# Attention scores of the last step, moved behind the next group of turns

## The chip, the cores and the metric

The kernel runs on one core of a Trainium2 chip. The metric is the device time of one execution in microseconds (us), from inputs in the chip's memory to the output in it. A core has a matrix engine (TensorE, in the rows PE for its matmuls and PEld for its weight loads), a vector engine (VectorE, DVE), a scalar engine (ScalarE, ACT), GpSimd (POOL) and an engine that issues transfers (SyncE, SP). Each of them runs its own instructions in the order in which the program gives them, and waits on semaphores for the others.

## What is computed

An attention layer, a dense layer pair and a routed layer pair, one after the other. The change lies in the attention, so its reference stands here; the other two follow on its output of 2304 x 512.

```python
batch, n_heads, seq, head_dim = (4, 8, 576, 64)

def _attn_ref(q, k, v):
    B, H, S, D = q.shape
    block = 64
    scores = (1.0 / np.sqrt(D)) * np.matmul(q, k.transpose(0, 1, 3, 2))
    pos = np.arange(S)
    mask = pos[:, None] // block >= pos[None, :] // block
    scores = np.where(mask, scores, -1000000000.0)
    scores = scores - np.max(scores, axis=-1, keepdims=True)
    attn = np.exp(scores)
    attn = attn / (np.sum(attn, axis=-1, keepdims=True) + 1e-09)
    return np.matmul(attn, v).astype(np.float32)
```

## The kernel before

The 32 heads are worked on in 16 pairs (`PAIRS`, index `u`), two heads side by side in the 128 partitions. The 576 rows of a head are nine blocks of 64; block `i` needs the first `64*(i+1)` keys. The nine blocks of a pair are taken in four steps, `STEPS = [(8, 5), (4, 3), (7, 6), (2, 1, 0)]`. Steps 0 and 2 use the first two banks of the score memory `s_ps`, steps 1 and 3 the other two, so that step `n` may be written only when the exponentials of step `n - 2` have read theirs.

For one step the engines do this in turn:

- PE `score(u, j)`: the products of queries and keys (L1320, 64 rows by 64 columns of the array, two heads at a time).
- DVE `most(u, j)`: the largest score of each row, one reduction per block (L902). It waits for `scored`.
- ACT `exp(u, j)`: the exponentials with their row sums, one ACTIVATE per block (L703). It waits for `maxed`.
- DVE `invert(u, j)`: adds 1e-9 to the row sums (L907), takes the reciprocal (L909) and, for steps 0 to 2, multiplies the step's first block (L914). It waits for `exped` of the whole step. POOL `normalise(u, j)` multiplies the other blocks (L558).
- PE `turn_first(u, j)` and `turn_second(u, j)`: transposes of the probabilities (L1291), the first into the bank `a_ps`, the second into `d_ps`.
- ACT `first_out(u, j)` (L684) copies `a_ps` and DVE `second_out(u, j)` (L896) copies `d_ps` into `pt`. Each of the two banks holds one group of turns at a time: the next group into `d_ps` waits for `dve_free`, the next into `a_ps` for `act_free`.
- PE `weigh_many(u, ...)` and `weigh_few(u)`: the products with the values (L1342), the second for blocks 0 to 3. ACT `many_x` and `few_x` (L684) copy them out.

The rows of keys and queries of pair `u + 1` are turned by `turn_keys` and `turn_queries` (L1273) through the same two banks, and copied out by `keys_out` on ACT and `queries_out` on DVE (L888).

The order on each engine is written out by hand in a loop over `u`, and pairs overlap: while the scores of pair `u` are made, the last two steps of pair `u - 1` are turned and weighed. On PE one round of the loop is: scores 0 of `u`; turns of step 2 of `u - 1`; scores 1; first part of keys and queries of `u + 1`; first part of `weigh_many(u - 1)`; turns of step 3 of `u - 1`, mixed with the rest of keys and queries; scores 2; rest of `weigh_many(u - 1)`; turns of step 0 of `u`; scores 3; `weigh_few(u - 1)`; turns of step 1. On DVE a round begins with `invert(u - 1, 3)`, which stands in front of `most(u, 0)`, `second_out(u - 1, 2)` and `most(u, 1)`. In the last round there are no keys and queries to turn; after it PE turns step 2 of pair 15, waits for the exponentials of its step 3 (their banks are needed), and starts on the dense layers (`hidden`, L1372), whose first inputs `x_hi` and `x_lo` come from ACT (L684) and DVE (`split_x`, L924, queued behind `invert(15, 3)`).

Of the kernel before, what the change touches and what calls it, by code (L numbers as in the profile page):

```python
# [27 lines left out]
def routed_transformer_block(  # L28
# [101 lines left out]
    def blocks_before(u, j):  # L130

        return NB * u + sum(len(c) for c in STEPS[:j])
# [147 lines left out]
    with ctx:  # L280
# [74 lines left out]
        def scores(i):  # L355
            return s_ps[:, SCORE_AT[i]:SCORE_AT[i] + BLK * (i + 1)]
# [6 lines left out]
        def x_at(u):  # L363
            return u % PPB * TOK + u // PPB * SEQ
# [317 lines left out]
        def _(act):  # L682
            def high(dst, src):
                return act.activation(dst, src, ACT.Copy)  # L684


            def keys_out(u, n):
                act.wait_ge(act_full, A_TURN["k", u, n])
                high(kt[:, u % 2, TURNED[n]:TURNED[n + 1]],
                     a_ps[:, TURN_AT[n]:TURN_AT[n] + TURNED[n + 1] - TURNED[n]]).then_inc(act_free, 1)  # L690

            def first_out(u, j):
                cs = first_turn(j)
                at = slot(cs[0][0], 0)

                act.wait_ge(act_full, A_TURN["k", u + 2, 1] if j == 3 and u + 2 < PAIRS else A_TURN["p", u, j])
                high(pt[:, u % 2, at:at + len(cs), :].rearrange("p c n -> p (c n)"), a_ps[:, 0:P * len(cs)]).then_inc(act_free, 1)

            def exp(u, j):
                for m, i in enumerate(STEPS[j]):  # L700

                    act.wait_ge(maxed, blocks_before(u, j) + {8: 2, 1: 3}.get(i, m + 1))
                    act.activation(probs[:, PROB_AT[i]:PROB_AT[i] + BLK * (i + 1)], scores(i), ACT.Exp,  # L703
                                   bias=neg_max[:, i:i + 1], accum_out=row_sum[:, j, m:m + 1]).then_inc(exped, 1)
# [5 lines left out]
            def few_x(u):  # L710
                act.wait_ge(few_done, u + 1)
                high(x_t[:, x_at(u):x_at(u) + BLK * FEW], o_few).then_inc(few_out, 1)
# [15 lines left out]
            for u in range(PAIRS):  # L728
                more = u + 1 < PAIRS
                if u > 0:  # L730
                    first_out(u - 1, 2)
                exp(u, 0)
                if more:
                    keys_out(u + 1, 0)
                exp(u, 1)
                if u > 0:
                    first_out(u - 1, 3)
                if more:
                    keys_out(u + 1, 1)
                else:  # L740

                    act.wait_ge(dve_full, D_TURN["q", u, 1])
                    split_x(0, parts=range(0, 2))
                exp(u, 2)
                if u > 0:
                    many_x(u - 1)
                first_out(u, 0)
                exp(u, 3)
                first_out(u, 1)
                if u > 0:  # L750
                    few_x(u - 1)
            u = PAIRS - 1
            first_out(u, 2)
            split_x(0, parts=range(2, KC))
# [122 lines left out]
        def _(dve):  # L877
# [13 lines left out]
            def second_out(u, j):  # L891
                cs = second_turn(j)
                at = [slot(i, c) for i, c, _ in cs]
                step = at[1] - at[0]
                dve.wait_ge(dve_full, D_TURN["q", u + 2, 1] if j == 3 and u + 2 < PAIRS else D_TURN["p", u, j])
                dve.tensor_copy(pt[:, u % 2, at[0]:at[-1] + 1:step, :],  # L896
                                d_ps[:, 0:P * len(cs)].rearrange("p (c n) -> p c n", n=P)).then_inc(dve_free, 1)

            def most(u, j):
                dve.wait_ge(scored, NST * u + j + 1)  # L900
                for i in STEPS[j]:
                    dve.tensor_reduce(neg_max[:, i:i + 1], scores(i), AX_X, ALU.max, negate=True).then_inc(maxed, 1)  # L902

            def invert(u, j):
                n = len(STEPS[j])
                dve.wait_ge(exped, exps(u, j))
                dve.tensor_scalar(row_sum[:, j, 0:n], row_sum[:, j, 0:n], 1e-9, None, ALU.add).then_inc(summed, 1)  # L907
                dve.wait_ge(summed, NST * u + j + 1)
                dve.reciprocal(row_inv[:, j, 0:n], row_sum[:, j, 0:n]).then_inc(inverted, 1)  # L909
                if j < NST - 1:  # L910
                    dve.wait_ge(inverted, NST * u + j + 1)
                    i = STEPS[j][0]
                    p = probs[:, PROB_AT[i]:PROB_AT[i] + BLK * (i + 1)]
                    dve.tensor_scalar(p, p, row_inv[:, j, 0:1], None, ALU.mult).then_inc(long_normed, 1)  # L914
# [13 lines left out]
            for u in range(PAIRS):  # L928
                more = u + 1 < PAIRS
                if u > 0:  # L930
                    invert(u - 1, 3)
                most(u, 0)
                if u > 0:
                    second_out(u - 1, 2)
                most(u, 1)
                if more:
                    queries_out(u + 1, 0)
                invert(u, 0)
                if u > 0:
                    second_out(u - 1, 3)  # L940
                    if more:
                        queries_out(u + 1, 1)
                most(u, 2)
                if more and u == 0:
                    queries_out(u + 1, 1)
                invert(u, 1)
                second_out(u, 0)
                most(u, 3)
                invert(u, 2)
                second_out(u, 1)  # L950
            invert(PAIRS - 1, 3)

            dve.wait_ge(few_out, PPB)
# [302 lines left out]
        def _(pe):  # L1256
# [46 lines left out]
            def turn_second(u, j):  # L1303
                dve_bank(D_TURN["p", u, j])
                pe.wait_ge(short_normed, pool_normed(u, j))
                turn_probs(j, second_turn(j), d_ps).then_inc(dve_full, 1)

            def score(u, j):

                n = NST * u + j  # L1310
                if n >= 2:
                    pe.wait_ge(exped, exps((n - 2) // NST, (n - 2) % NST))
                if j == 0:
                    pe.wait_ge(act_free, A_TURN["k", u, 1])
                    pe.wait_ge(dve_free, D_TURN["q", u, 1])
                def product(m, i, lo, hi):
                    for h in range(2):
                        own = slice(BLK * h, BLK * h + BLK)
                        g = h if m == 0 else 1 - h
                        mm = pe.matmul(scores(i)[BLK * g:BLK * g + BLK, lo:hi], qt[own, u % 2, BLK * i:BLK * i + BLK],  # L1320
                                       kt[own, u % 2, lo:hi], start=True, stop=True, skip_group_check=True)
                    return mm

                if j == 0:

                    product(1, 5, 0, BLK * 6).then_inc(five_scored, 1)
                    product(0, 8, 0, 512)
                    pe.wait_ge(five_scored, u + 1)
                    mm = product(0, 8, 512, SEQ)
                else:  # L1330
                    for m, i in enumerate(STEPS[j]):
                        mm = product(m, i, 0, BLK * (i + 1))
                mm.then_inc(scored, 1)
# [84 lines left out]
            for u in range(PAIRS):  # L1418
                more = u + 1 < PAIRS
                score(u, 0)  # L1420
                if u > 0:
                    turn_first(u - 1, 2)
                    turn_second(u - 1, 2)
                score(u, 1)
                if more:
                    turn_keys(u + 1, 0)
                    turn_queries(u + 1, 0)
                if u > 0:
                    weigh_many(u - 1, (0, 1))
                    turn_first(u - 1, 3)  # L1430
                    if more:
                        turn_keys(u + 1, 1)
                    turn_second(u - 1, 3)
                    if more:
                        turn_queries(u + 1, 1)
                score(u, 2)
                if more and u == 0:
                    turn_keys(u + 1, 1)
                    turn_queries(u + 1, 1)
                if u > 0:  # L1440
                    weigh_many(u - 1, (2, 3, 4))
                turn_first(u, 0)
                turn_second(u, 0)
                score(u, 3)
                if u > 0:
                    weigh_few(u - 1)
                turn_first(u, 1)
                turn_second(u, 1)
            u = PAIRS - 1
            turn_first(u, 2)  # L1450
            turn_second(u, 2)
# [192 lines left out]
```

## Time and profile before

| | us |
|---|---|
| median of 3 runs | 793.68 |
| lowest and highest | 793.31 and 795.92 |
| the profiled execution | 793.63 |
| its span in the profile | 791.9 |

The profiled execution took 793.63 us, 1.7 us more than its span; that remainder lies outside the instructions. PE is counted busy in 98% of the span, DVE in 63%, ACT in 37%, POOL in 32%. The attention takes the first 190 us, the dense layers come next, and the routed layers last. The granted clock of TensorE is given in shares of 2.4 GHz.

In a row of the timeline the columns are: start in us, busy us, engine, line, operation, what is written and what is read, form and count; in brackets the idle time of the engine just before and who ended it. Rows of the same form that follow each other are merged, and the us are then those of all of them together.

### The profile page before, as it was taken

To read this page: it belongs to the slowest core of one execution; us is meant where nothing else is said; L and a number is where in the kernel's file an instruction comes from. 1 tells how busy PE (TensorE), PEld (TensorE's weight loads), DVE (VectorE), ACT (ScalarE), POOL (GpSimd) and SP (SyncE) were. 2 spreads that over 40 slices of the span, in tenths; PEclk is the share of its full clock that TensorE was granted. 3 is DMA by queue.
4 is the path that set the end of the run, shared out by engine and by line. 5 is a ranking of instruction groups with operands and counts; after the bars stand their busy time and mean duration, and the time that the engine had idled before them with its cause. 6 is when DMAs were issued, how large, how long until landed. Compare 5 with 4: busy or idle time off the path is not lost.

```text
span 791.9 us, 14922 instructions
## 1 busy us (share of the span) xinstructions
PE 774.8 (98%) x4600; PEld 605.9 (77%) x4601; DVE 501.6 (63%) x1242; ACT 296.3 (37%) x738; POOL 252.0 (32%) x307
## 2 busy tenths in 40 slices
PE   5999999999999999999999999999999999999996
PEld 3565556555888888888888888888998888888885
DVE  4887888876543376665766566654558565666653
ACT  3676767675101121113011220112217264555642
POOL 4767677776870000002000200002131223333333
PEclk9999999999999999999999999999999999999999
DMA  8243454321337330001000010000172376655564
GB/s 183 75 99 92 103 118 113 87 72 36 109 78 2 53 122 0 1 1 54 0 0 0 0 54 1 0 1 1 54 192 88 123 241 203 201 211 193 178 212 148
DMA packets 88154, 69.27 MB, mean 87 GB/s; under 512 B 66962, under 2 KB 66962, under 8 KB 88104
## 3 DMA queue, kind: packets, MB, share of 16 engines
q1 hardware_dynamic: 83160, 62.93, 29.7%
q0 software_dynamic: 3760, 5.38, 2.1%
q8 instruction: 30, 0.49, 0.3%
q10 hardware_dynamic: 1184, 0.30, 0.2%
q14 instruction: 20, 0.16, 0.1%
HBM read 62.97 MB, written 8.84 MB: 91 GB/s over the span
## 4 chain that ended last, share of the span: by engine, by line
PE 73%; DMA 14%; issue 5%; DVE 3%; POOL 2%; POOLq 1%; SPq 0%; DVEq 0%
PE psum L1372 50%; DMA xg<-out_dram,rec_next 8%; PE psum L1320 7%; PE psum L1342 6%; PE psum L1291 6%; DMA out_dram<-y_rows,rec_now 4%; PE psum L1273 2%; DMA out_dram<-y_rows,rec_early 2%; POOL rec_next L629 1%; PE psum L1468 1%; DMA q_rows<-in_q_dram 1%; DVE neg_max L902 1%; DVE we L1219 1%; POOLq L395 0%; POOL probs L558 0%
## 5 line engine op out<-in xcount | busy, mean ns | idle before, releaser
L800 ACT ACTIVATE g<-psum 128x512 f32<-128x512 f32 (+1 forms) x80 | 44.5, 556 | 306.8 <-PE psum L1372 306.8
L1106 DVE TENSOR_TENSOR g<-psum,g 128x512 f32<-128x512 f32 (+1 forms) x80 | 51.0, 638 | 157.6 <-ACT g L800 157.4
L583 POOL DMA_INDIRECT lists<-rec,slot_i x18 | 19.2, 1069 | 331.5 <-DVE slot_i L1040 327.5
L558 POOL TENSOR_SCALAR probs<-probs,row_inv 128x384 f32<-128x384 f32 (+2 forms) x96 | 99.0, 1042 | 57.1 <-DVE row_inv L909 57.1
L1372 PE MATMUL psum<-x_hi,wi_hi 128*128 128x512 f32 x256 | 100.1, 391 | 0.0
L1372 PE MATMUL psum<-x_hi,wi_lo 128*128 128x512 f32 x256 | 99.7, 389 | 0.0
L1372 PE MATMUL psum<-x_lo,wi_hi 128*128 128x512 f32 (+1 forms) x256 | 99.6, 389 | 0.0
L703 ACT ACTIVATE probs<-psum,neg_max 128x576 f32<-128x576 f32 (+2 forms) x144 | 74.6, 526 | 34.4 <-DVE neg_max L902 33.0
L1136 DVE TENSOR_TENSOR we<-w_half,we x96 | 59.0, 685 | 33.3 <-ACT we L684 33.3
L1372 PE MATMUL psum<-wo_hi,g_hi 128*128 128x512 f32 x192 | 74.9, 390 | 0.1
L1372 PE MATMUL psum<-wo_lo,g_hi 128*128 128x512 f32 x192 | 74.7, 389 | 0.0
L1372 PE MATMUL psum<-wo_hi,g_lo 128*128 128x512 f32 x192 | 74.7, 389 | 0.0
L684 ACT ACTIVATE we<-w_half (+1 forms) x112 | 60.1, 620 | 30.9 <-PE psum L1559 27.7
L902 DVE TENSOR_REDUCE neg_max<-psum 128x1 f32<-128x576 f32 (+2 forms) x144 | 62.9, 484 | 13.5 <-PE psum L1320 13.4
L1554 PE MATMUL psum<-we,xe_hi 128*128 (+1 forms) x240 | 61.0, 396 | 0.0
L1320 PE MATMUL psum<-kt,qt 64*64 64x64 f32 (+7 forms) x640 | 59.7, 435 | 0.8 <-DVE qt L888 0.5
L1579 PE MATMUL psum<-we,he_hi 128*128 (+1 forms) x240 | 58.8, 397 | 0.5 <-DVE y_rows L1202 0.5
L1342 PE MATMUL psum<-pt,v_rows 128*64 128x320 f32 (+4 forms) x448 | 56.1, 370 | 0.4 <-DVE pt L896 0.4
L1110 DVE TENSOR_TENSOR g_lo<-g,g_hi 128x512 fp32r<-128x512 f32 (+1 forms) x80 | 54.7, 683 | 2.8
L1372 PEld LDWEIGHTS psum<-x_hi,wi_lo 128*128 128x128 f32 x256 | 48.1, 188 | 10.1
L1372 PEld LDWEIGHTS psum<-x_hi,wi_hi 128*128 128x128 f32 x256 | 48.1, 188 | 10.0 <-issue 0.2
L1372 PEld LDWEIGHTS psum<-x_lo,wi_hi 128*128 128x128 f32 x256 | 48.1, 188 | 9.8
(229 smaller groups left out, 1486.7 us busy)
## 6 DMA issues: line engine op xcount, KB each, us to landing
w_half<-in_moe_w_dram SPq DMA_DIRECT2D x64, 512.0 KB, 3.8
q_rows<-in_q_dram SPq DMA_DIRECT2D x32, 144.0 KB, 3.0
out_dram<-x_rows SPq DMA_DIRECT2D x18, 256.0 KB, 2.1
k_rows<-in_k_dram SPq DMA_DIRECT2D x30, 144.0 KB, 3.2
v_rows<-in_v_dram SPq DMA_DIRECT2D x32, 128.0 KB, 2.3
w_raw<-in_moe_w_in_dram SPq DMA_DIRECT2D x16, 256.0 KB, 3.5
w_raw<-in_moe_w_out_dram SPq DMA_DIRECT2D x16, 256.0 KB, 2.6
wide_x<-w_rows SPq DMA_DIRECT2D x4, 256.0 KB, 5.3
```

The source lines that it names most:

```text
L558: pool.tensor_scalar(p, p, row_inv[:, j, m:m + 1], None, ALU.mult).then_inc(short_normed, 1)
L684: return act.activation(dst, src, ACT.Copy)
L703: act.activation(probs[:, PROB_AT[i]:PROB_AT[i] + BLK * (i + 1)], scores(i), ACT.Exp, bias=neg_max[:, i:i + 1], accum_out=row_sum[:, j, m: ...
L902: dve.tensor_reduce(neg_max[:, i:i + 1], scores(i), AX_X, ALU.max, negate=True).then_inc(maxed, 1)
L1106: dve.tensor_tensor(g_f, h_at(f, first, last), g_f, ALU.subtract).then_inc(g_done, 1)
L1110: dve.tensor_tensor(g_at(g_lo, f, last), g_f, g_at(g_hi, f, last), ALU.subtract).then_inc(g_lo_done, 1)
L1136: ins = dve.tensor_tensor(lo, w_half[:, bass.ds(h % 2, 1), cols].rearrange("p o n -> p (o n)"), hi, ALU.subtract)
L1320: mm = pe.matmul(scores(i)[BLK * g:BLK * g + BLK, lo:hi], qt[own, u % 2, BLK * i:BLK * i + BLK], kt[own, u % 2, lo:hi], start=True, stop=T ...
L1342: mm = pe.matmul(dst[own, :], v_rows[0:k, u % 2, c, own], pt[0:k, u % 2, at:at + step * (n - 1) + 1:step, own], start=first, stop=last, sk ...
L1372: mm = pe.matmul(dst, w, m, start=(first and n == 0), stop=(last and n == 2), skip_group_check=True)
L1554: pe.matmul(dst, xe_hi[:, kk, :], weights(h, part, F2 * kk + 512 * n), start=(kk == part == 0), stop=False, skip_group_check=True)
L1579: pe.matmul(y_ps, he_hi[:, t, :], weights(h, part, DM * t), start=(t == part == 0), stop=False, skip_group_check=True)
```

## The change

The group of step 3 (its scores on PE, its row maxima on DVE, its exponentials on ACT) is moved for all pairs but the first. On PE it stood between the turns of step 0 and `weigh_few`; now it stands behind the turns of step 1, directly in front of the next round's scores 0. On DVE `most(u, 3)` moves behind `invert(u, 2)` and `second_out(u, 1)`, directly in front of the next round's `invert(u, 3)`. On ACT `exp(u, 3)` moves behind `first_out(u, 1)` and `few_x(u - 1)`, directly in front of the next round's `first_out(u, 2)`. POOL's and SP's code is as before, and no instruction is added or taken away.

```diff
@@ ACT
                 first_out(u, 0)
-                exp(u, 3)
+                if u == 0:
+                    exp(u, 3)
                 first_out(u, 1)
                 if u > 0:
                     few_x(u - 1)
+                    exp(u, 3)
@@ DVE
                 second_out(u, 0)
-                most(u, 3)
+                if u == 0:
+                    most(u, 3)
                 invert(u, 2)
                 second_out(u, 1)
+                if u > 0:
+                    most(u, 3)
@@ PE
                 turn_second(u, 0)
-                score(u, 3)
-                if u > 0:
+                if u == 0:
+                    score(u, 3)
+                else:
                     weigh_few(u - 1)
                 turn_first(u, 1)
                 turn_second(u, 1)
+                if u > 0:
+                    score(u, 3)
```

PE before, from the turns of step 0 of a pair to the next pair's first scores (L1291 turns, L1320 scores, L1342 products with the values):

```order
L1291 MATMUL psum<-ident,probs 128x128 x4
L1291 MATMUL psum<-swap,probs 128x128 x3
L1291 MATMUL psum<-ident,probs 64x128
L1320 MATMUL psum<-kt,qt 64x192 x2
L1320 MATMUL psum<-kt,qt 64x128 x2
L1320 MATMUL psum<-kt,qt 64x64 x2
L1342 MATMUL psum<-pt,v_rows 64x256 x2
L1342 MATMUL psum<-pt,v_rows 64x128 x2
L1291 MATMUL psum<-ident,probs 128x128 x3
L1291 MATMUL psum<-swap,probs 128x128 x2
L1320 MATMUL psum<-kt,qt 64x384 x2
L1320 MATMUL psum<-kt,qt 64x512 x2
```

The same place after the change (lines are five higher):

```order
L1296 MATMUL psum<-ident,probs 128x128 x4
L1296 MATMUL psum<-swap,probs 128x128 x3
L1296 MATMUL psum<-ident,probs 64x128
L1347 MATMUL psum<-pt,v_rows 64x256 x2
L1347 MATMUL psum<-pt,v_rows 64x128 x2
L1296 MATMUL psum<-ident,probs 128x128 x3
L1296 MATMUL psum<-swap,probs 128x128 x2
L1325 MATMUL psum<-kt,qt 64x192 x2
L1325 MATMUL psum<-kt,qt 64x128 x2
L1325 MATMUL psum<-kt,qt 64x64 x2
L1325 MATMUL psum<-kt,qt 64x384 x2
L1325 MATMUL psum<-kt,qt 64x512 x2
```

The scores of 192, 128 and 64 columns, those of step 3, now stand next to the scores of 384 and 512 columns, those of the next pair's step 0.

DVE before, from the copy of step 0's turns to the copy of step 2's turns in the next round (the reductions x3 are step 3's, those x2 the next pair's step 0):

```order
L896 COPY pt<-psum 128x512
L902 TENSOR_REDUCE neg_max<-psum 128x1 x3
L907 TENSOR_SCALAR row_sum<-row_sum 128x2
L909 RECIPROCAL row_inv<-row_sum 128x2
L914 TENSOR_SCALAR probs<-probs,row_inv 128x512
L896 COPY pt<-psum 128x256
L907 TENSOR_SCALAR row_sum<-row_sum 128x3
L909 RECIPROCAL row_inv<-row_sum 128x3
L902 TENSOR_REDUCE neg_max<-psum 128x1 x2
L896 COPY pt<-psum 128x512
```

The same place after the change (lines are two higher):

```order
L898 COPY pt<-psum 128x512
L909 TENSOR_SCALAR row_sum<-row_sum 128x2
L911 RECIPROCAL row_inv<-row_sum 128x2
L916 TENSOR_SCALAR probs<-probs,row_inv 128x512
L898 COPY pt<-psum 128x256
L904 TENSOR_REDUCE neg_max<-psum 128x1 x3
L909 TENSOR_SCALAR row_sum<-row_sum 128x3
L911 RECIPROCAL row_inv<-row_sum 128x3
L904 TENSOR_REDUCE neg_max<-psum 128x1 x2
L898 COPY pt<-psum 128x512
```

Step 3's three reductions now stand directly in front of L909 on three columns, which waits for the exponentials of the same step.

## Rows read from the trace of the kernel before

**Rows 1.** The page, busy time of each engine, and the chain that ended last.

```profile
PE 774.8 (98%) x4600; PEld 605.9 (77%) x4601; DVE 501.6 (63%) x1242; ACT 296.3 (37%) x738; POOL 252.0 (32%) x307
...
PE 73%; DMA 14%; issue 5%; DVE 3%; POOL 2%; POOLq 1%; SPq 0%; DVEq 0%
```

**Rows 2.** Busy time in one round (stretch; PE, PEld, DVE, ACT, POOL; clock, DMA, GB/s).

```profile
107.06:118.22 11.16, 11.16 (x110) 6.61 (x106) 9.07 (x27) 7.97 (x27) 7.96 (x9) 1.00 0.44 104
```

**Rows 3.** Chain that ended last, same round (start us, us, what): PE's own pieces.

```profile
107.13 1.02 PE psum L1291 x8
108.15 0.49 PE psum L1320 x8
108.64 0.80 PE psum L1342 x8
109.44 0.70 PE psum L1291 x5
110.14 1.19 PE psum L1320 x12
111.33 1.02 PE psum L1291 x8
112.36 0.69 PE psum L1320 x6
```

**Rows 4.** Timeline of PE, scores of step 3, and the first query turn.

```profile
108.08 0.56 PE L1320 MATMUL psum<-kt,qt 64*64 64x192 f32 x12
...
113.36 0.25 PE L1273 MATMUL psum<-ident,q_rows 96*128 96x96 f32 x1
```

**Rows 5.** Timeline of DVE, same round.

```profile
108.19 0.69 DVE L896 COPY pt<-psum 128x512 f32<-128x512 f32 x1 [0.34 <-PE psum L1291]
108.80 0.68 DVE L902 TENSOR_REDUCE neg_max<-psum 128x1 f32<-128x192 f32 x3
...
110.18 0.42 DVE L896 COPY pt<-psum 128x256 f32<-128x256 f32 x1
110.52 0.27 DVE L907 TENSOR_SCALAR row_sum<-row_sum 128x3 f32<-128x3 f32 x1
110.82 0.18 DVE L909 RECIPROCAL row_inv<-row_sum 128x3 f32<-128x3 f32 x1
111.38 1.22 DVE L902 TENSOR_REDUCE neg_max<-psum 128x1 f32<-128x576 f32 x2 [0.39 <-PE psum L1320]
112.52 0.68 DVE L896 COPY pt<-psum 128x512 f32<-128x512 f32 x1
```

**Rows 6.** Timeline of ACT, first exponential of step 3 and its last row sum.

```profile
109.18 0.42 ACT L703 ACTIVATE probs<-psum,neg_max 128x192 f32<-128x192 f32 x1 [0.31 <-DVE neg_max L902]
...
110.13 0.20 ACT L703 ACTIVATION_READ_ACCUMULATOR probs<-psum,neg_max 128x1 f32 x1
```

**Rows 7.** Timeline of DVE, the round of pair 1.

```profile
21.61 0.18 DVE L909 RECIPROCAL row_inv<-row_sum 128x3 f32<-128x3 f32 x1
21.70 0.73 DVE L902 TENSOR_REDUCE neg_max<-psum 128x1 f32<-128x576 f32 x1
```

**Rows 8.** Timeline, last round: copy of DVE, products of PE.

```profile
179.46 0.68 DVE L896 COPY pt<-psum 128x512 f32<-128x512 f32 x1
...
180.40 0.49 PE L1342 MATMUL psum<-pt,v_rows 128*64 128x320 f32 x2 [0.42 <-DVE pt L896]
```

**Rows 9.** Timeline of POOL, four blocks of steps 2 and 3.

```profile
109.84 3.44 POOL L558 TENSOR_SCALAR probs<-probs,row_inv 128x448 f32<-128x448 f32 x4 [1.20 <-DVE row_inv L909]
```

**Rows 10.** Timeline of PE and DVE, behind the last round.

```profile
188.26 0.18 DVE L909 RECIPROCAL row_inv<-row_sum 128x3 f32<-128x3 f32 x1
188.38 0.69 DVE L924 TENSOR_TENSOR x_lo<-x_t,x_hi 128x512 fp32r<-128x512 f32 x1
...
188.21 0.66 PE L1291 MATMUL psum<-ident,probs 128*128 128x128 f32 x4 [0.63 <-ACT pt L684]
189.51 0.47 PE L1372 MATMUL psum<-x_hi,wi_hi 128*128 128x512 f32 x1
```

## The prediction

> **What bounds the kernel now.** I read the page first. TensorE is busy in 98% of the span and carries 73% of the chain that ended last; VectorE is busy in 63% [rows 1]. The change touches only the rounds of the attention, so the next view is one round. The stretch from one pair's turns of step 0 to the next pair's is 11.16 us; PE is busy in all of it at a granted clock of 1.00 (2.4 GHz), DVE in 9.07 us of it [rows 2]. The chain in that stretch consists of PE pieces that touch each other, with no other engine between them [rows 3]. So PE's own work sets the round, and the others just keep up. What has to be asked of a new order is whether they still do. DVE has about 2 us to spare in a round, but it works in order, so the sum of its work says little; the waits at its head decide.
>
> I count in us behind the start of the turns of step 0, which is 107.06 in rows 2 and in the timeline (the chain counts to ends and runs 0.07 later [rows 3]). Before the change PE stands like this: scores 3 at 1.02, `weigh_few` at 1.51, turns of step 1 at 2.31, scores 0 of the next pair at 3.01, turns of step 2 at 4.20, scores 1 at 5.23 (the slots of [rows 3], added up), and the first query turn at 113.36 - 107.06 = 6.30 [rows 4].
>
> The query turn is the place to watch. It writes the bank that the turns of step 2 used, and so it waits for DVE's copy of them. That copy ends at 112.52 + 0.68 - 107.06 = 6.14 [rows 5], just 0.16 before the query turn starts at 6.30. This wait is hidden today, with almost nothing over.
>
> **The change part by part.**
>
> *PE.* No matmul is added. `weigh_few` now starts at 1.02 and takes 0.80, the turns of step 1 start at 1.82 and take 0.70, and scores 3 start at 2.52 in place of 1.02. Scores 3 take 0.49 before [rows 3], though their columns need less: 192 + 128 + 64, twice each, is 768 columns, which at 2.4 GHz is 0.32. The other 0.17 is what going from one kind of matmul to another costs at the group's two ends. Scores 3 now meet scores 0, which are of the same kind, while `weigh_few` still stands between two groups of turns, so one such passage falls away. I value it at 0.10 and bound it by 0 and 0.17. Scores 0 then start at 2.91 and the turns of step 2 at 4.10. Without a wait, scores 1 would start at 5.13 and the query turn at 6.20.
>
> *DVE, up to the maxima.* Behind the copy of step 0's turns (from 1.13 [rows 5]) come `invert(u, 2)` and the copy of step 1's turns. In the profile all this with the maxima of step 3 took from 108.19 to 110.60, 2.41; without their 0.68 it is 1.73, which ends at 2.86, or at about 3.0 since step 1's turns end near 2.6. The maxima of step 3 wait for the scores: 2.52 + 0.56 [rows 4] = 3.08, and DVE starts some 0.06 later, at 3.14. So DVE's earlier work is no burden there.
>
> *ACT.* The first exponential of step 3 starts 109.18 - 108.80 = 0.38 behind the first of the maxima [rows 5, 6], at 3.52. From there to the end of the last row sum are 110.33 - 109.18 = 1.15 [rows 6], so the exponentials end at 4.67. The copies that ACT now does before, of the turns of step 1 and of `weigh_few`, are over by then: both inputs are ready 0.5 and more before 3.5.
>
> *DVE, the new wait.* Before the change `invert(u, 3)` came to the head of DVE at 110.52, when the exponentials had ended at 110.33: it waited for nothing. Now it stands directly behind the maxima on which those exponentials depend. DVE finishes the maxima at 3.14 + 0.68 = 3.82 and stands still until 4.67. Behind the waiting instruction are queued the maxima of scores 0, the copy of step 2's turns and the maxima of scores 1, and PE waits for that copy. Its time: `row_sum` at 4.71, the reciprocal 0.30 later (110.52 to 110.82 [rows 5]) at 5.01, the maxima of step 0 another 0.09 later at 5.10. That last step is from the round of pair 1, where the scores were there already [rows 7]; in the later rounds DVE waited for PE between them. From the first of these maxima to the copy are 112.52 - 111.38 = 1.14 [rows 5], so the copy runs from 6.24 to 6.92.
>
> *PE, the stall.* The query turn comes after the copy's end. How long after, one row shows for another instruction: in the last round the products of L1342 started 180.40 - (179.46 + 0.68) = 0.26 behind the copy [rows 8], but with further waits in between. The query turn carries the wait itself, so I take 0.10, between 0 and 0.26. It starts at 7.02, where before it was 6.30: 0.72 later. From there to the end of the round all is as before, PE and DVE both being late by about the same. The saved passage does not lessen this, for it lies behind the start of scores 3, inside the time that PE now spends waiting. Each round therefore gets some 0.72 longer, 11.16 to about 11.88.
>
> *How often.* Scores 3 are late for pairs 1 to 15. The stall at the query turn appears in the rounds of pairs 2 to 14, 13 times: 13 x 0.72 = 9.4. In the round of pair 15 there are no queries; there the products of L1342 wait for the same copy today already [rows 8], so its delay of 6.92 - 6.14 = 0.78 is passed on whole: 0.8. Behind that round the first matmul of the dense layers needs `x_lo`, which DVE makes behind `invert(15, 3)`. The reciprocal stood 3.76 behind the round's turns of step 0 in the round shown [rows 5] and comes at 5.01 now, 1.25 later. `x_lo` started 0.12 behind it and took 0.69 [rows 10], so it would be there at 5.82 in place of 4.57; PE began with it 0.44 behind its end (189.51 against 189.07 [rows 10]), and of these I leave 0.1, which makes PE 0.9 later: 0.9.
>
> *What is free.* POOL's normalising of step 2 begins earlier, since `invert(u, 2)` no longer stands behind the maxima. Step 3's begins behind the reciprocal, at about 5.2, and its three short blocks take some half of the row's 3.44 for four [rows 9]; they end near 7.0, and the turns that need them come only behind the query turns and the first products with the values. Nothing is added to any queue of transfers. The dense and routed layers follow on the attention and start later by the whole amount; PE is the bound there too [rows 1], so nothing of it comes back.
>
> *The sum.* 9.4 + 0.8 + 0.9 = 11.1 us on the profiled execution's 793.63, that is 804.7. That execution stands at the median of 793.68, so the forecast is 804.8.
>
> **The rivals.** *Only the saved passage counts.* If the new wait on DVE were covered, PE would gain 0.10 in each of 15 rounds, 1.5 us: 792.2; with the upper bound of 0.17 it would be 791.1, which is faster by just over 0.3%. This decides itself at one point: from the start of scores 3 to the end of the copy my chain takes 6.92 - 2.52 = 4.40, and 3.58 would be needed to be in time for a query turn at 6.20. For that the exponentials' whole latency seen by DVE, 4.67 - 3.82 = 0.85, would have to vanish. For it speaks only that PE has no slack, so that any passage saved counts at once; against it speak all the rows of the chain above. The Trainium skill speaks for this rival's gain: TensorEngine Tiling (Array Packing), in Key Properties, says that changing the tiling mode drains the engine. By that rule putting two groups of one mode together must save time on PE; the 0.17 above agrees with it, and the page gives no price.
>
> *A part of the stall.* If PE restarts at once, the passage between `weigh_few` and the turns is cheaper than in the row, and DVE's `row_sum` on three columns is shorter once the copy in front of it is gone, a round loses about 0.35: 13 x 0.35 + 1.3 = 5.9, 799.5.
>
> *A longer chain.* If ACT takes up the exponentials 0.4 later, because its copies now stand in front of them, scores 1 begin to wait too (they have 5.13 - 4.67 = 0.46), and each round loses 1.1: 13 x 1.1 + 2.5 = 16.8, 810.4. The rows give ACT 8 busy us in 11 [rows 2], so this is unlikely.
>
> **How the numbers follow.** The forecast has 0.86, the rival with only the saved passage 0.05, a part of the stall 0.05, the longer chain 0.04. Within the forecast a round loses 0.53 at least (restart at once, passage 0.1 cheaper) and 0.98 at most (restart 0.26, passage 0.1 dearer): 13 x 0.53 + 1.5 = 8.4 and 13 x 0.98 + 2.0 = 14.7, so 802.1 to 808.4. With a little of the second rival the range is 801.5 to 808.5. About 0.3%, 2.4 us, is what a measurement of this kernel can tell from no change. Slower by more: 0.95; within it 0.03; faster by more 0.02.
>
> **What would show it.** The round should be near 11.9 us, alike in all rounds from pair 2 on. DVE should show idle time of about 0.9 in front of L907 (now L909) on three columns, released by the exponentials, and no longer any in front of the maxima of scores 0. PE should show idle time or a gap of some 0.8 in front of the first query turn, released by the copy into `pt`. Between scores 3 and scores 0 no gap should be left. I would be wrong if the round kept 11.0 to 11.2, or if PE's gap stood in front of scores 1 instead.

## The result

| | us |
|---|---|
| before, median of 4 runs (lowest, highest) | 793.55 (793.31, 795.92) |
| changed kernel, median of 4 runs (lowest, highest) | 806.79 (804.01, 808.18) |
| changed over before | 1.0152, 95% interval 1.0132 to 1.0171 |
| the changed kernel's profiled execution, its span | 808.18, 806.5 |

The change makes the kernel 1.5% slower, 13.2 us between the medians; 804.8 was forecast, with 801.5 to 808.5. A second set of 6 runs of the same kernel gave 804.99 (804.30 to 806.38) against 794.49, a ratio of 1.0125 (1.0104 to 1.0146). The difference between the sets is told of below.

In the page of the changed kernel PE's busy time has hardly risen, while its share of a longer span has fallen from 98% to 96% (compare [rows 1]). In the chain that ended last DVE has twice its former share, 6% in place of 3%, and ACT, which had none, has 2%:

```profile
PE 778.3 (96%) x4600; PEld 605.9 (75%) x4601; DVE 502.8 (62%) x1242; ACT 297.8 (37%) x738; POOL 250.8 (31%) x307
...
PE 75%; DMA 10%; DVE 6%; issue 4%; ACT 2%; POOL 2%; POOLq 1%; DVEq 0%; SPq 0%
```

One round, from the turns of step 0 of one pair to those of the next, answers to [rows 2] (same columns):

```profile
112.01:123.86 11.85, 11.27 (x109) 6.55 (x106) 9.08 (x27) 8.07 (x27) 7.97 (x9) 1.00 0.41 98
```

It takes 11.85 us where it took 11.16, PE is busy in 11.27 of it, and the other engines do what they did. The clock is 1.00 in both. The chain that ended last shows where the time is; it is the view of [rows 3], for the changed kernel (start us, us, what):

```profile
112.07 1.02 PE psum L1296 x8
113.10 0.80 PE psum L1347 x8
113.90 0.74 PE psum L1296 x5
114.64 0.56 PE psum L1325 x8
115.20 0.02 issue
115.22 0.37 DVE neg_max L904
115.59 0.02 issue
115.62 1.17 ACT probs L703 x6
116.78 0.02 issue
116.81 0.18 DVE row_sum L909
116.99 0.02 issue
117.01 0.18 DVE row_inv L911
117.19 1.11 DVE neg_max L904 x2
118.30 0.61 DVE pt L898
118.90 0.04 issue
118.95 0.55 PE psum L1278 x4
```

Before, this chain was PE from end to end. Now it leaves PE at the end of scores 3, goes over the first maximum, the six ACT instructions of three exponentials, the row sums and their reciprocal, the maxima of scores 0 and the copy into `pt`, and comes back to PE at the query turn. Two rows of the timeline name the two places where an engine stands still, DVE in front of the row sums (0.90) and PE in front of the query turn (0.58):

```profile
116.81 0.17 DVE L909 TENSOR_SCALAR row_sum<-row_sum 128x3 f32<-128x3 f32 x1 [0.90 <-ACT probs L703]
...
118.95 0.38 PE L1278 MATMUL psum<-ident,q_rows 96*128 96x96 f32 x2 [0.58 <-DVE pt L898]
```

### The profile page after: what moved, and what is told of

It is laid out like the page before. It is cut to its first block, busy times and chain, and to the rows that moved or that the text cites. A ratio compares the mean times of both kernels' runs of the same rounds, so it can differ in the third digit from the quotient of the medians.

```text
span 806.5 us, 14922 instructions
## 1 busy us (share of the span) xinstructions
PE 778.3 (96%) x4600; PEld 605.9 (75%) x4601; DVE 502.8 (62%) x1242; ACT 297.8 (37%) x738; POOL 250.8 (31%) x307
## 4 chain that ended last, share of the span: by engine, by line
PE 75%; DMA 10%; DVE 6%; issue 4%; ACT 2%; POOL 2%; POOLq 1%; DVEq 0%; SPq 0%
PE psum L1377 46%; PE psum L1347 7%; PE psum L1296 5%; DMA xg<-out_dram,rec_next 4%; PE psum L1562 4%; PE psum L1325 4%; DMA out_dram<-y_rows,rec_now 3%; PE psum L1587 3%; DVE neg_max L904 3%; ACT probs L703 2%; PE psum L1278 2%; PE psum L1567 2%; PE psum L1592 2%; DVE pt L898 1%; DMA xg_third<-out_dram,rec_early 1%
## 5 line engine op out<-in xcount | busy, mean ns | idle before, releaser
L583 POOL DMA_INDIRECT lists<-rec,slot_i x18 | 19.2, 1067 | 331.3 <-DVE slot_i L1045 327.4
L904 DVE TENSOR_REDUCE neg_max<-psum 128x1 f32<-128x576 f32 (+2 forms) x144 | 62.6, 482 | 10.8 <-PE psum L1325 8.9
L1325 PE MATMUL psum<-kt,qt 64*64 64x512 f32 (+7 forms) x640 | 57.6, 436 | 0.8 <-DVE qt L890 0.5
```

## The experiments

### The same kernel again

```diff
(no edit to the changed kernel)
```

> The changed kernel, unaltered, a second profile and more times. In its first profile the first matmul of the dense layers is 10.8 us later than before, and the routed layers begin with a wait of 3.2 us for the third early gather, which the kernel before does not show. Theory: the rounds of the attention take 11.85 us in every execution, and the first matmul of the dense layers is again 10.8 to 10.9 us late; the wait for the gather comes and goes, so that the times spread from 804 (without) to 808 (with). Rival: the wait for the gather belongs to the changed order, is there in every profile with 3 us, and the time stays near 807 to 808.

Measured: 804.99 (804.30 to 806.38), ratio 1.0125. The rounds are again 11.85 to 11.86, and the first matmul of the dense layers comes at 199.91, 10.4 us later than before's 189.51 (10.8 in the first profile: the rounds of pairs 2 to 14 add 9.1 in both, the loading at the start differs by 0.4; counted from pair 1's turns of step 0 the delay is 10.8 in both). The routed layers begin without a wait, at 605.97. In the first profile they began with one:

```profile
609.81 0.66 PE L1506 MATMUL psum<-ident,xg_first 128*128 128x128 f32 x4 [3.20 <-DMA xg_third<-out_dram,rec_early]
```

So about 3 of the first profile's 14.6 us of longer span (806.5 against 791.9) are not the attention's. PE waited there for the third of three gathers of token rows that POOL starts ahead of the routed layers. That this wait comes and goes is shown; the rival, 3 us in every execution, has fallen. Whether the change makes the wait more frequent is not shown.

### The wait on DVE taken away: `invert` behind the copy

```diff
@@ DVE (on the changed kernel)
-                if u > 0:
-                    invert(u - 1, 3)
                 most(u, 0)
                 if u > 0:
                     second_out(u - 1, 2)
+                    invert(u - 1, 3)
```

> The changed kernel, with one more edit on DVE: invert of the last pair's step 3 stands behind the maxima of scores 0 and the copy of step 2's turns, no longer in front of them. Theory (the loss is DVE standing still in front of that invert while the maxima and the copy are queued behind it): the gap in front of the query turn goes, and the round falls from 11.85 to between 11.0 (11.16 less the 0.145 that scores 3 and scores 0 save by standing together) and 11.2 (if POOL, which normalises step 3 now 1.4 us later, makes the turns of step 3 wait 0.1 to 0.2). The time is 791 to 794. Rival (the loss comes from scores 3 standing late on PE, whatever DVE does): the round stays at 11.6 or more, and the time above 800.

Measured: 800.83 (798.70 to 803.82), ratio 1.0062 (1.0038 to 1.0085); the time expected was 791 to 794, so the theory missed it. The query turn no longer waits; it starts 0.39 behind the key turns. But the round is 11.39, neither the 11.0 to 11.2 of the theory nor the 11.6 of its rival. The rest stands at the second turns of step 3, which started 0.48 behind the key turns next to them, where before it was 0.17. Timeline of PE before:

```profile
115.28 0.33 PE L1273 MATMUL psum<-ident,k_rows 96*128 96x96 f32 x2
115.45 0.38 PE L1291 MATMUL psum<-swap,probs 128*128 128x128 f32 x2
```

Timeline of POOL and PE in this kernel:

```profile
115.65 1.29 POOL L558 TENSOR_SCALAR probs<-probs,row_inv 128x128 f32<-128x128 f32 x2
...
116.61 0.33 PE L1277 MATMUL psum<-ident,k_rows 96*128 96x96 f32 x2
117.09 0.41 PE L1295 MATMUL psum<-swap,probs 128*128 128x128 f32 x2
```

POOL's last multiplication of step 3 ends at 116.95 and PE goes on 0.14 later. Nearly half a microsecond of each round's loss (11.85 to 11.39) went with `invert` out of the way; moving `invert` back uncovered the next thing that was late, POOL's three blocks of step 3. The expectation had named it, at 0.1 to 0.2 in place of 0.31. The first matmul of the dense layers comes 4.4 us later than before: 3.0 in the 13 rounds and 1.6 behind them, less 0.2 in the loading. (This profile also has a gather wait of 3.73.)

### PE's part of the change undone

```diff
@@ PE (on the changed kernel)
-                if u == 0:
-                    score(u, 3)
-                else:
+                score(u, 3)
+                if u > 0:
                     weigh_few(u - 1)
                 turn_first(u, 1)
                 turn_second(u, 1)
-                if u > 0:
-                    score(u, 3)
```

> The changed kernel with PE's order as before: only the maxima and the exponentials of step 3 stand at their new places on DVE and ACT, and scores 3 are early. Theory (the wait in front of invert is made by the maxima and exponentials being behind the copy of step 1's turns, so PE's part does not matter for it): maxima at 3.46 us behind the round's turns of step 0, exponentials done at 4.99, copy of step 2's turns done at 7.24, query turn at 7.36 in place of 6.30; the round takes 12.2 and the time is 809 to 812. Rival (PE's late scores 3 are the cause): the round is 11.3 or less and the time under 796.

Measured: 810.51 (809.66 to 813.72), ratio 1.0204. The round is 12.09. With scores 3 early and only their maxima and exponentials late, it is slower still. Timeline of DVE:

```profile
116.81 0.68 DVE L904 TENSOR_REDUCE neg_max<-psum 128x1 f32<-128x192 f32 x3
118.38 0.17 DVE L909 TENSOR_SCALAR row_sum<-row_sum 128x3 f32<-128x3 f32 x1 [0.89 <-ACT probs L703]
118.58 0.18 DVE L911 RECIPROCAL row_inv<-row_sum 128x3 f32<-128x3 f32 x1
118.67 1.19 DVE L904 TENSOR_REDUCE neg_max<-psum 128x1 f32<-128x576 f32 x2
119.78 0.68 DVE L898 COPY pt<-psum 128x512 f32<-128x512 f32 x1
```

The round's turns of step 0 started at 113.35, so the maxima stand at 3.46, as expected, and the copy ends at 7.11 (7.24 expected). PE's late scores are not the cause; what costs is that the maxima, their exponentials and `invert` follow each other on DVE's queue with nothing between. It is slower than the changed kernel because the maxima start later, at 3.46 in place of 3.21: they stand behind DVE's copy of step 1's turns, and PE makes those turns later when scores 3 are in front of them.

### The chain shortened and lengthened

```diff
@@ ACT, exp(u, j) (on the changed kernel), one exponential for step 3
+                if u > 0 and j == 3:
+                    act.wait_ge(maxed, blocks_before(u, j) + 3)
+                    act.activation(probs[:, PROB_AT[2]:PROB_AT[2] + 3 * BLK], scores(2), ACT.Exp,
+                                   bias=neg_max[:, 2:3], accum_out=row_sum[:, j, 0:1]).then_inc(exped, 3)
+                    return
```

> The changed kernel with one exponential for step 3 in place of three, for all pairs but the first: blocks 1 and 0 of step 3 are left out, so the output is not the reference's, the routing of tokens may differ, and only the attention's rounds are to be read. The one exponential starts behind the last of the maxima, at 3.86 us behind the turns of step 0, and ends at 4.37 in place of 4.67. Theory (the query turn hangs on the end of the exponentials by a chain): the round gets 0.30 shorter, 11.55. Rival (the query turn hangs on PE's start of scores 3 and DVE's own work): the round stays at 11.85.

Measured: the round is 11.59, 0.26 shorter where 0.30 was expected, and DVE waits 0.64 in front of the row sums in place of 0.90. The whole kernel took 815.90; its tokens are routed otherwise, so that number says nothing on the change.

```diff
@@ ACT, exp(u, j) (on the changed kernel), four exponentials for step 3
+                if u > 0 and j == 3:
+                    act.wait_ge(maxed, blocks_before(u, j) + 1)
+                    act.activation(x2_rows[:, 0, 0:3 * BLK], scores(2), ACT.Exp, bias=neg_max[:, 2:3])
```

> The changed kernel with one exponential more in step 3 for all pairs but the first (block 2's scores are also written to a place that nothing reads then), in front of the three. Theory (a chain from scores 3 over the exponentials to the query turn, without slack): each round gets longer by the 0.32 that such an exponential holds ACT, 11.85 to 12.17, and the time is 4.5 to 5 us above the changed kernel's, 809. Rival (slack in the chain): the round stays under 12.0.

Measured: 811.01 (809.26 to 811.37), ratio 1.0211. The round is 12.17, 0.31 longer for an instruction that holds ACT for 0.32. DVE's wait, timeline of this kernel:

```profile
118.84 0.17 DVE L912 TENSOR_SCALAR row_sum<-row_sum 128x3 f32<-128x3 f32 x1 [1.21 <-ACT probs L706]
```

It grew from 0.90 to 1.21. The first matmul of the dense layers comes 4.6 us later than in after_again, as 15 late groups at 0.31 each would have it; the median is 2 us above the 809 expected. Both runs show a slope of one: each tenth of a microsecond on DVE's wait is a tenth on every round. There is no slack in this chain in either direction over these 0.3 us.

### The rest of the loss: one block from POOL to DVE

```diff
@@ (on invert_behind)
-    POOL_BLOCKS = [(5,), (3,), (6,), (2, 1, 0)]
+    POOL_BLOCKS = [(5,), (3,), (6,), (2, 1)]
@@ DVE, invert
-                if j < NST - 1:
-                    dve.wait_ge(inverted, NST * u + j + 1)
-                    i = STEPS[j][0]
-                    p = probs[:, PROB_AT[i]:PROB_AT[i] + BLK * (i + 1)]
-                    dve.tensor_scalar(p, p, row_inv[:, j, 0:1], None, ALU.mult).then_inc(long_normed, 1)
+                dve.wait_ge(inverted, NST * u + j + 1)
+                m = 0 if j < NST - 1 else 2
+                i = STEPS[j][m]
+                p = probs[:, PROB_AT[i]:PROB_AT[i] + BLK * (i + 1)]
+                dve.tensor_scalar(p, p, row_inv[:, j, m:m + 1], None, ALU.mult).then_inc(long_normed, 1)
@@ PE, turn_first, turn_second
-                    pe.wait_ge(long_normed, (NST - 1) * u + j + 1)
+                    pe.wait_ge(long_normed, NST * u + j + 1)
...
-                    pe.wait_ge(short_normed, pool_normed(u, j) - 2)
+                    pe.wait_ge(short_normed, pool_normed(u, j) - 1)
...
+                if j == NST - 1:
+                    pe.wait_ge(long_normed, NST * u + j + 1)
```

> As invert_behind, and DVE multiplies the last block of step 3 (64 columns) itself, so that POOL has two blocks of step 3 in place of three. In invert_behind the round was 11.39; the query turn no longer waited, but the second turns of step 3 started 0.39 behind the key turns in place of 0.08, 0.145 after POOL's last multiplication of step 3. Theory (that wait of 0.31 is all that is left of the change's loss): the round falls to 11.0 to 11.1, below the 11.16 of before, the first matmul of the dense layers comes 0 to 1.5 us earlier than before, and the time is 0 to 2 us below before's unless the early gather is waited for. Rival (DVE, which gets one instruction more in front of the maxima of scores 1, makes PE wait elsewhere): the round stays at 11.2 or more.

Measured: 794.25 (793.66 to 798.90), ratio 1.0010 (0.9995 to 1.0026). One round:

```profile
106.10:117.16 11.06, 11.06 (x110) 6.53 (x106) 9.78 (x28) 8.09 (x27) 7.64 (x8) 1.00 0.43 105
```

The theory holds for the round: 11.05, PE busy throughout, and 0.10 less than before's 11.16. It fails for the time, which is not below before's. The first matmul of the dense layers came at 189.20, 0.31 earlier than before, and 0.2 of that lies ahead of pair 1's turns, in the loading; 13 rounds at 0.10 to 0.11 promise 1.4. From pair 15's scores 0 to that matmul it took 13.82 us in place of 12.50:

```profile
189.20 0.47 PE L1378 MATMUL psum<-x_hi,wi_hi 128*128 128x512 f32 x1 [1.35 <-DVE x_lo L926]
```

### The last pair at its old place

```diff
@@ ACT, DVE and PE (on block0_dve); so for exp(u, 3), most(u, 3) and score(u, 3)
-                if u == 0:
-                    exp(u, 3)
+                if u in (0, PAIRS - 1):
+                    exp(u, 3)
...
-                if u > 0:
-                    exp(u, 3)
+                if 0 < u < PAIRS - 1:
+                    exp(u, 3)
```

> As block0_dve, and pair 15 keeps step 3 at its old place (as pair 0 does). In block0_dve the rounds took 11.05 in place of 11.16, but from the scores 0 of pair 15 to the first matmul of the dense layers it was 13.82 in place of 12.50. Theory (that 1.3 is the price of the late exponentials of the last pair, which no next pair's work covers): the stretch goes back to 12.4 to 12.6, the rounds stay at 11.05, the first matmul of the dense layers comes 1.4 to 1.7 us earlier than before, and the undisturbed times lie near 792. Rival: the stretch stays above 13 because DVE's extra instruction and the late invert make it long.

Measured: 793.26 (792.02 to 794.95), ratio 0.9989 (0.9980 to 0.9998). The rounds stay at 11.05, the first matmul of the dense layers comes at 187.59, 1.9 us earlier than before, and it no longer waits for `x_lo`. Of the 1.9 us 0.7 lie ahead of pair 1's turns of step 0, which start at 28.26 in place of 28.96; the kernel before had them at 28.26 too in another profile (before_clear), so this part is loading and not the order. The attention itself is 1.2 us shorter: 1.35 in the rounds, less 0.13 behind them. From pair 15's scores 0 to the dense layers it takes 12.68, just above the 12.4 to 12.6 expected; the rival, above 13, has fallen. The end of the stretch:

```profile
187.21 0.63 PE L1296 MATMUL psum<-swap,probs 128*128 128x128 f32 x4 [0.26 <-POOL probs L558]
187.59 0.48 PE L1379 MATMUL psum<-x_hi,wi_hi 128*128 128x512 f32 x1
```

The row of POOL's release is the one that before had at its end too, with the same 0.26; only the wait for `x_lo` is gone. Before:

```profile
189.12 0.63 PE L1291 MATMUL psum<-swap,probs 128*128 128x128 f32 x4 [0.26 <-POOL probs L558]
```

This version is faster than before by a tenth of a per cent, 0.8 us between the medians (before's is 794.04 in that set). That is of the size that the passage between scores 3 and scores 0 can give once every wait is covered, and too small beside the spread of the times to be told from it exactly.

### The early gathers and the weight loads

```diff
@@ SP (on the changed kernel, on the kernel before, and on last_old)
             load_half(0, 0, first)
+            sp.wait_ge(early_xg, 16 * EARLY)
             load_half(0, 1, first)
```

> The changed kernel; SyncE issues the second half of the first expert's weights only when the three early gathers have landed. In the profiles so far the eight loads of w_half and the wait for the third gather went together: 18.9 and 18.6 us of loading without a wait, 21.25 with 1.5, 23.4 with 3.2, 23.9 with 3.7. Theory (the gathers compete with the weight loads on the transfer engines): the gather lands 2 us or more before it is needed in every profile, and the times lie within 1 us of one another near 804, if the later half of the weights is still in time. Rival (the transfers are slow in some executions whoever else uses them): the spread of 2 to 4 us stays. A third outcome: the weights' second half comes late and costs up to 5 us.

> The kernel before with the same single wait on SyncE. Its times so far spread from 793.3 to 798.5. Theory: they close up near 793.5, and the distance to after_clear is 10.4 us, the delay that the rounds of the attention alone make. Rival: the spread stays. Third outcome as in after_clear.

> As last_old, with SyncE's wait for the early gathers in front of the second half of the first expert's weights. In before_clear 12 times lay between 792.8 and 794.05, where before's 23 lay between 792.9 and 798.2. Theory: the times lie within 1.3 us near 791.8, 0.3% under before's median of 794.3. Rival: the gathers' wait returns, since after_clear still spread over 2.4 us.

Measured: on the changed kernel 805.70 (804.30 to 806.69), ratio 1.0143 (1.0120 to 1.0165); on the kernel before 793.35 (792.80 to 794.05, 12 runs), ratio 0.9986 (0.9973 to 0.9999), beside 23 runs of before without the edit from 792.87 to 798.22; on last_old 792.45 (792.11 to 793.58, 11 runs), ratio 0.9985 (0.9976 to 0.9994), beside before's 793.25 to 795.79. For last_old with this edit 791.8 and a spread of 1.3 were expected, and both were missed a little (792.45 and 1.5). Beside last_old without it, in the same set, the median is 0.8 lower and the spread half as wide, so the gain over before is here the order's and this edit's together. None of the three profiles has a gather wait, nor a wait of PE above 0.7 us for the weights that were held back.

In the profiles without the edit the eight loads of `w_half` took the longer, the longer PE waited for the gather: 18.3 to 19.2 us in the six profiles with no wait, 21.25 with 1.53 (pe_back), 23.41 with 3.20 (the first profile) and 23.92 with 3.73 (invert_behind). First the kernel before, whose routed layers began without a wait, then the changed one, timeline of SP:

```profile
575.66 18.90 SPq L488 DMA_DIRECT2D w_half<-in_moe_w_dram  x8
```

```profile
586.68 23.41 SPq L488 DMA_DIRECT2D w_half<-in_moe_w_dram  x8
```

On the kernel before, 23 runs without and 12 with the edit speak for the theory, that gathers and weights compete: the spread closes from 5.3 us to 1.3. On the changed kernel the 5 times still spread over 2.4 us, and the theory's 1 us fell there. The distance between the two medians is 12.4, not 10.4, though the first matmul of the dense layers is 11.2 us apart in their profiles (0.6 of it ahead of pair 1's turns) and the last one 11.3. What moves the changed kernel's undisturbed-looking times by up to 2 us stays open; no trace shows it, since the profile of after_clear fell on one of its fastest times.

## Why the prediction was right

*What bounds, and the place to watch.* Right. The query turn was named as the place, the copy of step 2's turns as what it waits for, and the chain of the changed kernel runs over just those steps.

*The positions.* In us behind the round's turns of step 0 (112.01), forecast and measured: scores 3 at 2.52 and 2.56 (`weigh_few` has a slot of 0.84 in place of 0.80 when turns stand on both sides); the first maximum at 3.14 and 3.21; the first exponential at 3.52 and 3.61; the end of the exponentials at 4.67 and 4.77; the maxima of scores 0 at 5.10 and 5.09; the end of the copy at 6.92 and 6.88; the query turn at 7.02 and 6.94. The two larger misses cancel: the early part, 0.10 too short, and the row sums, which were priced at the 0.27 of [rows 5] and took 0.17, so that the reciprocal follows in 0.20, not 0.30. Three smaller ones follow: from the first of the maxima to the copy 1.11 in place of 1.14, from the copy's end to PE 0.06 in place of 0.10, and behind the query turn 0.05 more, where nothing was forecast, since the four query turns take 0.48 after the stop where they took 0.42 without one. The query turn is thus 0.64 late and the round 0.70 longer, against 0.72 and 0.72. That the round came out at 11.85, against 11.88, is the right chain and some luck in its sizes. PE's gap is 0.58 and not "some 0.8": without the wait the query turn would have started at 118.21, 0.74 earlier, but the row counts from the end of the last key turn, 118.37.

*The passage saved.* Scores 3 and scores 0 together take 1.54, from 114.57 to the next turns, where apart they took 0.49 + 1.19 = 1.68 [rows 3]: 0.14 saved, within the bounds of 0 and 0.17. As forecast, it does nothing in the changed kernel, since it lies inside PE's wait; with the waits covered it shows as 0.10 a round (11.16 to 11.05), for `weigh_few` gives 0.04 of it back. The drain on a change of tiling mode that the Trainium skill states (TensorEngine Tiling (Array Packing), Key Properties) is a rule that agrees with this. No run here parts a drain from whatever else a passage costs; what is measured is the 0.14 for both.

*The count and the last round.* 13 rounds at 0.70 are 9.1, against 9.4. The last round and the stretch to the dense layers were forecast at 1.7 and took 1.75: from pair 15's scores 0 to the first matmul of the dense layers 14.24 in place of 12.50. The attention's whole delay was forecast at 11.1 and is 10.8 in both profiles, counted from pair 1's turns of step 0 (10.4 and 10.8 with the loading). This part is shown, by the chain, by the slope of one in both directions, and by the two kernels that take it away.

*What was not in the sum.* The forecast is 2.0 us under the first median and 0.2 under the second set's. The 0.2 is luck in part: before's median stood 0.9 higher in that set, and the distance there is 10.5 against the 11.1 forecast. In the first set it is 13.2. What the sum left out is the hand-over to the routed layers: "nothing of it comes back" was right, but PE is not the only bound there. The third gather is needed almost at once when it lands, and an execution in which it is late pays for it, 1.5 to 3.7 us in three profiles. The kernel before has late executions too (its times reach 798.5, and holding the loads back closes their spread), so the wait is not put down to the change, though no profile of before shows it. Why the changed kernel's first four times lie so far above before's is not settled by so few; the lowest of the two sets, 804.01 and 793.31, are 10.7 apart, which is the attention's delay.

*The rivals.* The rival with only the saved passage gave 792.2 and named the condition, a chain shorter by 0.8. In last_old that condition was met by moving `invert` out of the chain, and the median is 793.3 beside 794.0 for before, a gain of 0.8 where the rival had 1.5. The rival of a part of the stall (799.5) had two of its three terms right, PE's quick restart and the shorter row sums, and was still wrong: these are worth 0.14 a round where it needed 0.37, and the early part took 0.10 back. The rival of a longer chain (810.4) did not come: ACT took up the exponentials 0.40 behind the maxima, against the 0.38 forecast.

## What to carry to other kernels

Before moving a group of dependent work to a later place in hand-written orders, look at what stands directly behind it on each in-order engine: an instruction that needs the round trip to another engine blocks everything queued behind it. Here DVE stood still for 0.90 and each round paid 0.70, since the copy queued behind it used to end only 0.16 before it was needed. DVE's busy share of 63% doesn't show that; the distance of 0.16 does. A passage saved on the busiest engine counts only if every wait of the new order is covered; here three more edits were needed to turn a loss of 11 us into a gain of about 1. And the last turn of a pipelined loop has no next turn to hide behind, so it may want another order than the rest.

## What the runs showed of the hardware

How long DVE's row-sum instruction takes goes with what POOL does beside it. On 128 x 3 values it took 0.27 in all 16 pairs of the kernel before [rows 5], each time while POOL was multiplying a block of 448 columns. It took 0.17 in the 15 late rounds of the changed kernel, with DVE idle before it, and 0.16 in 15 rounds of invert_behind, directly behind a copy; in all of these POOL stood still. So the copy in front of it, which the prediction held for the reason, is not enough to make it long. On two values it takes 0.16 in most rounds, but in block0_dve it took 0.63 and 0.30 in nearly every round, where it began during an instruction of POOL and ended 0.02 behind that one's end. The first of the two, POOL and DVE:

```profile
105.45 1.27 POOL L551 TENSOR_TENSOR wi_lo<-w_raw,wi_hi 128x512 fp32r<-128x512 f32 x1
...
106.12 0.63 DVE L909 TENSOR_SCALAR row_sum<-row_sum 128x2 f32<-128x2 f32 x1
```

It is not so beside every instruction of POOL: in invert_behind the row sums on two values took 0.16 in the midst of a multiplication of 128 columns. What decides stays open. In block0_dve it cost nothing, since PE was busy throughout the round.

On PE a group of matmuls of one kind that stands between two groups of another takes about 0.14 more than next to its own kind: that is 44% of the 0.32 that the columns of scores 3 need at 2.4 GHz.
